# The expert stage as one engine loop over a ring of weight slots

## What is computed

```python
def _attn_ref(q, k, v):                      # (4, 8, 576, 64) each
    scores = scale * np.matmul(q, k.transpose(0, 1, 3, 2))
    gamma = 1.0 - 2.0 ** (-5.0 - np.arange(H))
    Dmat = np.where(rel >= 0, gamma[:, None, None] ** rel[None, :, :], 0.0)
    return np.matmul(scores * Dmat[None], v)
def _moe_ref(x, w_gate, w1, w2, capacity):   # x (2304, 512), E = 8, F = 1024, capacity 576
    logits = x @ w_gate
    expert_idx = np.argmax(logits, axis=1)
    gate_w = probs[np.arange(N), expert_idx]     # softmax of the logits
    # the tokens of an expert, in order, up to its capacity, fill disp[e]
    h = np.maximum(np.einsum('ecd,edf->ecf', disp, w1), 0.0)
    y = np.einsum('ecf,efd->ecd', h, w2)
    # out[i] = gate_w[i] * y[expert_idx[i], pos[i]], zero for what was not kept
```

## Time and profile before

| | us |
|---|---|
| median of 3 runs | 528.02 |
| lowest, highest | 526.66, 532.65 |
| span of the profiled execution | 525.8 |
| TensorE busy (products) | 424.8 |
| VectorE busy | 213.8 |
| ScalarE busy | 177.2 |

### The profile page before, as it was taken

How to read it: one execution, slowest core, us unless ns; L and a number is a source line. 1 busy time by engine, 2 the same in 40 slices (tenths; PEclk the granted TensorE clock), 3 DMA queues, 4 the chain that set the end, 5 groups by cost and what they waited for, 6 DMA issues and landing times.

```text
span 525.8 us, 9287 instructions
## 1 busy us (share of the span) xinstructions
PE 424.8 (81%) x3493; PEld 400.5 (76%) x3494; DVE 213.8 (41%) x410; ACT 177.2 (34%) x311; POOL 163.5 (31%) x155
## 2 busy tenths in 40 slices
PE   7999999979999779489539927963993990997980
PEld 4998999979986369489539927963993990997980
DVE  1364564554555336435405422640451461354210
ACT  2554333322521035145116303610630640452301
POOL 4444334354410340611602141160224224103302
PEclk9999999985979789889959977995896997798996
DMA  9989988765513125724605451570453453242101
GB/s 179 233 215 239 221 211 198 198 157 110 130 46 112 40 67 149 216 80 130 191 21 144 129 150 56 158 200 19 129 167 126 131 175 108 82 145 68 46 5 40
DMA packets 80952, 68.59 MB, mean 130 GB/s; under 512 B 62459, under 2 KB 62683, under 8 KB 80833
## 3 DMA queue, kind: packets, MB, share of 16 engines
q1 hardware_dynamic: 73344, 52.92, 37.8%
q0 software_dynamic: 6144, 9.46, 6.0%
q10 hardware_dynamic: 1344, 4.72, 2.9%
HBM read 57.62 MB, written 18.87 MB: 145 GB/s over the span
## 4 chain that ended last, share of the span: by engine, by line
PE 68%; issue 15%; DVE 6%; DMA 5%; POOL 2%; ACT 1%; SPq 1%; POOLq 0%; ACTq 0%; DVEq 0%
PE bank L574 13%; PE bank L576 13%; PE bank L575 13%; PE bank L451 6%; PE bank L439 3%; PE bank L434 3%; PE bank L421 3%; PE bank L467 3%; PE bank L410 3%; PE bank L594 3%; DMA w_raw<-in_moe_w 3%; DVE w_lo L801 2%; DMA k_raw<-in_k 2%; PE bank L564 2%; PE bank L461 1%
## 5 line engine op out<-in xcount | busy, mean ns | idle before, releaser
L574 PE MATMUL bank<-xs_hi,w_hi 128*128 128x288 f32 (+5 forms) x256 | 86.4, 337 | 72.0 <-issue 69.2
L574 PEld LDWEIGHTS bank<-xs_hi,w_hi 128*128 128x128 f32 x256 | 54.9, 215 | 75.8 <-issue 75.8
L367 POOL DMA_INDIRECT x_gat<-x_rows,slot_row x48 | 53.8, 1120 | 138.7 <-PE bank L564 82.2
L801 DVE TENSOR_TENSOR w_lo<-w_raw,w_hi 128x1024 fp32r<-128x1024 f32 x64 | 80.3, 1255 | 14.8 <-ACT w_hi L677 13.4
L374 POOL DMA_INDIRECT out<-y_nat,slot_row x48 | 46.1, 960 | 128.1 <-ACT y_nat L742 115.1
L576 PE MATMUL bank<-xs_lo,w_hi 128*128 128x288 f32 (+5 forms) x256 | 82.9, 324 | 1.2 <-issue 1.2
L575 PE MATMUL bank<-xs_hi,w_lo 128*128 128x288 f32 (+5 forms) x256 | 83.1, 325 | 0.0
L987 DVE SCALAR_TENSOR_TENSOR h_lo<-bank,h_hi 128x304 fp32r<-128x304 f32 (+5 forms) x64 | 29.4, 463 | 131.1 <-ACT h_hi L757 126.5
L677 ACT ACTIVATE w_hi<-w_raw 128x1024 fp32r<-128x1024 f32 x64 | 67.7, 1057 | 31.4 <-DMA w_raw<-in_moe_w 30.9
L574 PE MATMUL bank<-h_hi,w_hi 128*128 128x288 f32 (+5 forms) x256 | 77.4, 302 | 0.0
L575 PE MATMUL bank<-h_hi,w_lo 128*128 128x288 f32 (+5 forms) x256 | 76.4, 299 | 0.0
(11 more groups left out here) (93 smaller groups left out, 573.4 us busy)
## 6 DMA issues: line engine op xcount, KB each, us to landing
w_raw<-in_moe_w SPq DMA_DIRECT2D x64, 512.0 KB
q_raw<-in_q SPq DMA_DIRECT2D x24, 192.0 KB, 3.2
k_raw<-in_k SPq DMA_DIRECT2D x24, 192.0 KB, 4.0
v_raw<-in_v SPq DMA_DIRECT2D x24, 192.0 KB, 3.9
x_rows<-x_nat SPq DMA_DIRECT2D x24, 192.0 KB, 3.6
out<-zeros ACTq DMA_DIRECT2D x12, 384.0 KB, 3.1
x_gat<-x_rows,slot_row POOLq DMA_INDIRECT x48
out<-y_nat,slot_row POOLq DMA_INDIRECT x48, 2.8
```

Source lines behind the costliest of these rows:

```text
L367: pool.indirect_dma_start(out=x_gat[:, g, :], out_offset=None, in_=x_rows[:, :], in_offset=bass.IndirectOffsetOnAxis(ap=slot_row[:, g, e:e ...
L574: pe.matmul(dst[:, 0:n], w_hi, m_hi, start=(i == 0), stop=False)
L801: dve.tensor_tensor(lo, w_raw[i % 2][:, :], hi.bitcast(f32), ALU.subtract).then_inc(w_lo_made, 1)
```

## The change

On every engine the expert stage becomes one loop over the eight experts. Weights have eight raw buffers, and `w1_hi`, `w1_lo` four slots and `w2_hi`, `w2_lo` two, half an expert; a slot is filled again as soon as the product that read it has its result. The host lays out w1 and w2 so that each piece is one contiguous block per partition. On TensorE a body holds half of the up-products (or of the down-products) of one size and runs twice; there is a tree over the sizes for up and one for down, and the turning of x and y stands between them. Sizes are 256 to 336, 384 and the wide form for more. ScalarE and VectorE have two bodies, up to 384 columns and more. Groups are of 128 rows, three and two instead of four and two of 96. Some semaphores start at constants (`COPIED0` and so on) so that waits on registers stay positive. Core of the diff:

```diff
+G = 128
+NA = 3
+NG = -(-CAP // G)
-SIZES = [256, 272, 288, 304, 320, 336, 352, 384]
+SIZES = [256, 272, 288, 304, 320, 336, WA]
+FS, DS = FC // 2, DC // 2
...
-        w_raw = [sb(f"w_raw{i}", [128, F]) for i in range(2)]
+        w_raw = [sb(f"w_raw{i}", [128, F]) for i in range(PIECES)]
+        w1_hi = sb("w1_hi", [128, FS, DC, 128], f32r)
+        w2_hi = sb("w2_hi", [128, DS, FC, 128], f32r)
...
                 if i < 4:
+                    wait(sp, w1_lo_made, (e - 1) * FC + 2 * i + 2)
+                    sp.dma_start(w_raw[i][:, :], w1[e, i]).then_inc(w_in[i], 16)
                 else:
+                    wait(sp, w2_lo_made, (e - 1) * DC + i - 3)
+                    sp.dma_start(w_raw[i][:, :], w2[e, i - 4]).then_inc(w_in[i], 16)
...
-            load_weights(0, 0)
-            load_weights(0, 1)
...
+                    if first:
+                        load_weights(0, c)
+                    if last and c < PIECES - NC:
+                        load_weights(0, c + NC)
+            for e in range(1, E):
+                for i in range(PIECES):
+                    load_weights(e, i)
...
+            def up_all(e, n, wide):
+                with pe.Fori(0, 2) as it:
+                    for s in range(FS):
+                        pe.wait_ge(w1_lo_made, e * FC + it * FS + (s + 1))
+                        pe.wait_ge(result_copied, e * CHUNKS + it * (2, 2, 3, 4)[s] + ((-1, 0, 0, 0)[s] + COPIED0))
+                        last = up(ring[s][:, 0:n], s, slice(0, n))
...
+                        last.then_inc(result_made, 1)
+            def down_all(e, n, wide):
+                with pe.Fori(0, 2) as it:
+                    for s in range(DS):
+                        pe.wait_ge(w2_lo_made, e * DC + it * DS + (s + 1))
+                        pe.wait_ge(result_copied, e * CHUNKS + it * 4 + (FS + 1 + s) + COPIED0)
+                        def h_ready(f):
+                            pe.wait_ge(result_copied, e * CHUNKS + (f + 1) + COPIED0)
+                        last = down(ring[s][:, 0:n], s, slice(0, n), h_ready if s == 0 else None)
...
+                        last.then_inc(result_made, 1)
...
+            with pe.Fori(0, E) as e:
                 count = pe.value_load(counts[0:1, bass.ds(e, 1)], min_val=0, max_val=TOKENS)
+                pe.wait_ge(y_scaled, e * NA + (SCALED0 - NA))
...
+                pe.wait_ge(xs_lo_made, NA * (e + 1))
+                by_count(pe, count, lambda n, wide: up_all(e, n, wide))
+                with pe.If(e < E - 1):
+                    for g in range(NA):
+                        pe.wait_ge(gathered[g], 16 * (e + 2))
...
+                    for g in range(2):
+                        turn_x(x_banks[g], g).then_inc(xs_tr, 1)
+                with pe.If(e > 0):
+                    for g in range(2):
+                        turn_y(y_banks[g], g).then_inc(y_tr, 1)
...
+                by_count(pe, count, lambda n, wide: down_all(e, n, wide))
...
+            def expert(e, wide):
...
+                for f in range(FC):
+                    act.wait_ge(result_made, e * CHUNKS + (f + 1))
+                    last = act.activation(h_hi[:, f, 0:WA], ring[f % 4][:, 0:WA], ACT.Relu)
...
+                    last.then_inc(h_hi_made, 1)
+                    if f < FS:
+                        w1_high(e, f + FS)
+                    elif f < FS + DS:
+                        with act.If(e > 0):
+                            w2_high(e, f - FS)
...
+                for d in range(DS):
+                    act.wait_ge(result_made, e * CHUNKS + (FC + d + 1))
+                    w2_high(e, DS + d)
+                    with act.If(e < E - 1):
+                        w1_high(e + 1, 2 + d)
...
+                for f in range(FC):
+                    dve.wait_ge(h_hi_made, e * FC + (f + 1))
+                    last = h_low(ring[f % 4][:, 0:WA], f, slice(0, WA))
...
+                    last.then_inc(result_copied, 1)
+                    if f < FS:
+                        w1_low(e, f + FS)
+                    elif f < FS + DS:
+                        with dve.If(e > 0):
+                            w2_low(e, f - FS)
...
+                for d in range(DC):
+                    dve.wait_ge(result_made, e * CHUNKS + (FC + d + 1))
+                    last = dve.tensor_copy(y_sb[:, d, 0:WA], ring[d % 2][:, 0:WA])
...
+                    last.then_inc(result_copied, 1)
+                    if d < DS:
+                        w2_low(e, DS + d)
+                        with dve.If(e < E - 1):
+                            w1_low(e + 1, 2 + d)
```

More of the change, by code:

```diff
@@ L553, in _, with turn_x, turn_y, product @@
             keep_warm(4)
[L556 to L568, removed]
+            def turn_x(dst, g):
+                dst = dst.rearrange("p (a c) -> p a c", a=DC)
+                for d in range(DC):
+                    last = pe.transpose(dst[:, d, :], x_gat[:, g, d * 128:(d + 1) * 128], ident[:, :])
+                return last
+            def turn_y(dst, g, n=G):
+                for d in range(DC):
+                    last = pe.transpose(dst[0:n, d * 128:(d + 1) * 128], y_sb[:, d, g * G:g * G + n], ident[:, :])
+                return last
+            def product(dst, steps, before=None):
                 last = None
@@ L584, in down @@
-            def down(par, d, n, before=None):
-                cols = slice(d * 128, (d + 1) * 128)
-                return product(ring[d % 4], n, [(w2_hi[par][:, f, cols], w2_lo[par][:, f, cols],
-                                                 h_hi[:, f, 0:n], h_lo[:, f, 0:n]) for f in range(FC)], before)
-            def turn_y(e, g):
-                wait(pe, y_scaled, NA * e + g - 1)
-                for d in range(DC):
-                    last = pe.transpose(ytr_ps[g % 2][0:C, d * 128:(d + 1) * 128],
-                                        y_sb[:, d, g * C:(g + 1) * C], ident[:, :])
-                last.then_inc(y_tr, 1)
@@ new lines, in product, with up, down @@
+                    pe.matmul(dst, w_lo, m_hi, start=False, stop=False)
+                    last = pe.matmul(dst, w_hi, m_lo, start=False, stop=(i == len(steps) - 1))
+                return last
+            def up(dst, s, cols):
+                return product(dst, [(w1_hi[:, s, d, :], w1_lo[:, s, d, :], xs_hi[:, d, cols], xs_lo[:, d, cols])
+                                     for d in range(DC)])
+            def down(dst, s, cols, before=None):
+                return product(dst, [(w2_hi[:, s, f, :], w2_lo[:, s, f, :], h_hi[:, f, cols], h_lo[:, f, cols])
+                                     for f in range(FC)], before)
@@ L660, in _ @@
-            by_expert(pe, expert)
-            pe.wait_ge(result_copied, E * CHUNKS)
+                pe.wait_ge(y_scaled, e * NA + (SCALED0 - NA))
+                with pe.If(count <= WA):
+                    pe.sem_inc(b_xs_tr, NB)
+                with pe.Else():
+                    for g in range(NB):
+                        pe.wait_ge(gathered[NA + g], 16 * (e + 1))
+                        turn_x(wide_x[g], NA + g).then_inc(b_xs_tr, 1)
+                    pe.wait_ge(b_xs_lo_made, NB * (e + 1))
@@ new lines, in _, with by_columns @@
+            with dve.Fori(0, E) as e:
+                count = dve.value_load(counts[0:1, bass.ds(e, 1)], min_val=0, max_val=TOKENS)
+                with dve.If(count <= WA):
+                    expert(e, False)
+                with dve.Else():
+                    expert(e, True)
+def by_columns(w, together):
+    e, k, n = w.shape
+    a = w.reshape(e, k // 128, 128, n // 128 // together, together, 128)
+    return a.transpose(0, 3, 2, 4, 1, 5).reshape(e, n // 128 // together, 128, together * k)
```

488 lines of the change are left out of this document (224 added, 264 removed).

## The result

The changed kernel took 583.92 us (median of 4 runs, 582.8 to 587.25) against 529.2 of the kernel before beside it (4 runs, 526.66 to 532.65): a ratio of 1.108, with a 95% interval of 1.102 to 1.114. It is 11% slower, and far above the range of the prediction. The profiled execution has a span of 580.7 us against 525.8.

What follows compares the result with a forecast made beforehand. Fetches for far TensorE branches between experts were taken as the bound. Expert stage 209.6 + 18.5 + 48 + 12 + 3 = 291 us, 28.6 less; with 2.5 + 1.2 + 1.5 the gain is 33.8, giving 495 us, range 452 to 540.

Steps and rivals of the forecast that it cites:

- What bounds the kernel: Expert stage: TensorE idle 68.4 us in seven holes between experts, filled by long branches whose targets are fetched; half clock follows.
- (a): TensorE's arithmetic in the expert stage: products stay at 209.6 us, turning x and y takes 18.5 us, 3 us less.
- the bill: Expert stage before the change: counts of full-clock products per 5 us window, one per expert, giving 209.6 us of products.
- (c): Weights in the expert stage: DMA relaxed, splits just ahead of use tight; 0.4 us per expert, 3 us charged.
- The ring is late: Rival, chance 0.10: weight splits hold TensorE 2 us per expert more, 16 us, giving 511 us.
- (d): ScalarE and VectorE in the expert stage: always-384 columns add 0.1 us per step off the path; their branches cost nothing.
- (e): Start and end of the expert stage: 2.5 us less at the start, 1.2 us at the end.
- (f): Attention: two weight loads move behind the fourth chunk, last batch splits one piece on VectorE; 1.5 us gained of possible 5.
- The marks: Expected signs: stage 291 us, 12 to 15 long branches, fetches well below 51; wrong if long branches under 5 or over 20.
- All code stays: Rival, chance 0.18: TensorE keeps all expert-stage code after the first visit; stage 246 us, total 449 us.
- Two blocks only: Rival, chance 0.03: every far jump in the expert stage long, five or six per expert; stage 408 us, total 612 us.

Runs made afterwards that it cites:

- f3: Changed kernel with sizes 272, 304, 336, 384 and the first w2 piece split in the last batch's first chunk: 457.26 us, 0.859 of the kernel before.
- e3: Changed kernel with the first w2 piece split in the last batch's first chunk, not the first batch's last chunk: 582.47 us, 1.105 of the kernel before.
- g3: Changed kernel with sizes 272, 304, 336, 384 and its w2 split left where it was: 467.75 us, 0.889 of the kernel before.
- e2: Changed kernel with sizes 288, 336, 344, 352, 360, 368, 384, of which only two are picked: 474.25 us, 0.902 of the kernel before.
- f1: Changed kernel with five sizes, 272, 288, 304, 336, 384: 546.27 us.

## Why the prediction was wrong, step by step

**What bounds the kernel.** Right: the holes are fetches for far branches, half clock follows them. Kernels with 5 or 6 fetches in the stage have one of 256 to 264 us, those with 60 to 72 one of 369 to 389.

**(a) The work itself.** Right. In warm stretches of 5 us the changed kernel ran 42 products of 272 columns, 36 of 320, 35 of 336, 38 and 37 of 304, 40 and 39 of 288 and 44 of 256, each within one of the numbers of the bill. The sum for products and turning, 209.6 + 18.5 = 228.1 us, can stand.

```profile
q8 instruction: 11, 0.18, 1.5%
```

and the branches out of the up body, into the down body, out of it and back to the head take 3.28, 2.19, 6.22 and 4.46 us. Code that ran less than 50 us and some 360 instructions ago is fetched again, though the attention loop keeps 840 instructions.

The Trainium skill (Runtime: NRT & Kernel Launch, section Instruction fetch mechanics) calls the store a FIFO filled in blocks of 256 instructions. Its "Only 2 cache lines!" (Advanced Engine Details and Errata, section ISA Cache) is contradicted once more: with four sizes TensorE runs some 800 different instructions of a loop of 1,440, six experts long, without a fetch. The FIFO agrees with the cliff (72 fetches at six sizes, 6 at four). It agrees with the 11 fetches too: at 256 instructions each they bring in some 2,800, an estimate by that page, which is more than the whole loop. That the order of replacement is a FIFO's was not shown by itself.

**(c) The ring.** Right and even too dear: 3 us were charged, and TensorE waits nowhere for w_lo. "The ring is late" falls. It stays so when TensorE is fast: with four sizes the largest such wait is 0.7 us.

**(d) ScalarE and VectorE** at nothing: right in the changed kernel. It isn't quite nothing once the fetches are gone. With four sizes (f3) they are busy 39% and 50%, and TensorE waits between experts for VectorE's copy of the last y:

```profile
PE bank L567 <- DVE y_sb L1046: 5.6, 6, 1.1
```

In the changed kernel it waits 0.7 us for such a copy.

**(e) Entry and end.** The end gained 3.3 us where 1.2 were charged.

**(f) The attention. Wrong sign.** Entry and attention were to start the stage 4.0 us earlier, at 185.7; it started at 192.7. With the w2 split later it starts at 183.8 and 184.0 (e3, f3), so the terms were right and a wait was missing. (With the early split it starts between 191.9 and 198.2 in all kernels with that attention, so the 8 to 9 us stand clear of the difference between executions.) The first batch does run earlier, as said (the fourth chunk's last products at 29.1 us against 30.2), but behind it the first w2 split came only one chunk after its load, in a stretch with the DMA engines 88% busy. The prediction moved the loads and asked only what they were taken from; it never asked who uses them next and how far behind.

**The marks.** A stage of 291 us: no, 374.4. 12 to 15 long branches: 36, beyond the "over 20" that was to prove it wrong. Fetches well below 51: no, 68. Holes between up and down that weren't there: yes, 34.0 us. VectorE's wait on the path under 5 us: yes.

**The other rivals.** "All code stays" (stage 246, 449 us) is what the kernel is with four sizes: 257.5 to 259.4 and 457 to 468 us, with 19.9 us of holes in g3 where 12 were put and 5 us more of columns. "Two blocks only" (612 us) is close to six sizes in time, but with two blocks three sizes would be slow too.

## What to carry to other kernels

Before adding a specialised body to an engine's loop, count the instructions of the whole loop, over all the bodies that its rounds will visit, and treat what the engine keeps as a step: where most sizes were used, TensorE's loops here were free of fetches up to some 1,440 instructions and lost much or most of their code from some 1,660 on. Bodies that are never visited were free in one place (e2) and cost 75 us in another (f1), so measure. Four column sizes cost 5 us more of columns than seven and win by over 110 us. When a load is moved, look up the first instruction that reads it on every engine's queue and count the distance again.

## What the runs showed of the hardware

- In the changed kernel a branch into which a fetch fell took 2.2 to 7.2 us, mostly 2.9 to 4.5; 7.2 was one with two fetches, but others with two took 4.1 to 6.5. Seven of its 36 branches over 1 us hold no fetch and took 1.1 to 2.1 us. A branch to code that was kept took 0.06 to 0.4 us.
- TensorE went round a loop of about 1,440 instructions (four sizes, some 800 of them run) six times without a fetch, and round one of 2,100, of which 580 are run, as well. With some 1,880 (1,250 run) it made 72 fetches in eight rounds, and in the changed kernel 11 in a round that repeated the bodies of the round before.
- Code that is never run isn't always free: taking out the wide bodies at five sizes was worth 77.6 us (medians, 546.27 and 468.68).
- What stays open: how the store picks what it drops, how the placement of the bodies counts (six sizes were slower than seven), and why the stage of e3 took 9.5 us more than that of the changed kernel.
